# Score products of a retention kernel: one row tile per head, or four tiles of 64 by 64

## The reference, cut to what matters

```python
def _attn_ref(q, k, v):                       # B=2, H=8, S=768, D=64
    gamma = 1.0 - 2.0 ** (-5.0 - np.arange(H))
    for t in range(S):
        state = gamma * state + einsum('bhd,bhe->bhde', k[:, :, t], v[:, :, t])
        y[:, :, t] = scale * einsum('bhd,bhde->bhe', q[:, :, t], state)

def _moe_ref(x, U, V, w_ch1, w_ch2):          # x (2, 768, 512), rank 32
    u = x + ((x^T @ U @ V))^T                  # mixing over the tokens
    return u + relu(u @ w_ch1) @ w_ch2         # 512 -> 2048 -> 512

def _moe2_ref(x, w_in, w_spatial, b_spatial, w_out):
    h = relu(x @ w_in); u, v = halves of h
    v_n = v normalised over its 512 channels
    return (u * (w_spatial @ v_n + b_spatial)) @ w_out
```

## Time and profile before

| | us |
|---|---|
| median of three executions (464.69 to 465.3) | 465.14 |
| the profiled execution: its time | 464.75 |
| its span in the trace | 462.7 |
| PE busy | 456.1 (99%) |
| DVE busy | 351.2 (76%) |
| ACT busy | 253.6 (55%) |
| POOL busy | 48.4 (10%) |

### The profile page before, as it was taken

One profiled execution on the slowest core, in us unless ns is written; L12 is line 12 of the kernel. 1 busy time (PEld: TensorE's weight loads), 2 busy tenths in 40 slices (PEclk: granted clock), 3 DMA queues, 4 the chain that ended last, 5 costly groups with the idle time before them and its releaser, 6 DMA issues.

```text
span 462.7 us, 8760 instructions
## 1 busy us (share of the span) xinstructions
PE 456.1 (99%) x3176; PEld 407.9 (88%) x3176; DVE 351.2 (76%) x773; ACT 253.6 (55%) x592; POOL 48.4 (10%) x52
## 2 busy tenths in 40 slices
PE   8999999999999999999999999999999999999997
PEld 5788888999999999888888999988888789999997
DVE  4888879968889988864855976775722998895785
ACT  2676846456677555743474655643523675554352
POOL 2278960000000000000100000000100001000000
PEclk9999999999999999999999999999999999999999
DMA  8999601334342432211220333302105002032003
GB/s 310 408 316 349 243 1 47 136 138 137 136 141 87 145 118 93 93 37 55 92 91 3 102 135 120 101 1 92 47 0 204 1 0 93 0 124 104 1 1 136
DMA packets 20889, 51.36 MB, mean 111 GB/s; under 512 B 1520, under 2 KB 3952, under 8 KB 19568
## 3 DMA queue, kind: packets, MB, share of 16 engines
q1 hardware_dynamic: 20432, 50.29, 31.0%
q10 hardware_dynamic: 416, 0.53, 0.3%
HBM read 47.66 MB, written 3.15 MB: 110 GB/s over the span
## 4 chain that ended last, share of the span: by engine, by line
PE 88%; POOL 3%; DVE 3%; DMA 3%; ACT 1%; issue 1%; SPq 0%; DVEq 0%; POOLq 0%
PE bank L1632 10%; PE bank L1630 10%; PE bank L1633 9%; PE bank L1613 8%; PE bank L1611 8%; PE bank L1614 8%; PE bank L1737 3%; PE bank L1738 3%; PE bank L1735 3%; PE bank L1671 2%; PE bank L1672 2%; PE bank L1670 2%; PE bank L1753 2%; DMA tab<-decay 2%; PE bank L1518 1%; DMA att<-attn 1%
## 5 line engine op out<-in xcount | busy, mean ns | idle before, releaser
L1611 PE MATMUL bank<-bh,w1c 128*128 128x256 f32 x336 | 94.7, 282 | 0.1
L1614 PE MATMUL bank<-bh,w1c 128*128 128x256 f32 x336 | 94.7, 282 | 0.0
L1613 PE MATMUL bank<-bl,w1c 128*128 128x256 f32 x336 | 94.6, 282 | 0.0
L1632 PE MATMUL bank<-hl,w2h 128*128 128x512 f32 x192 | 75.9, 395 | 0.0
L1630 PE MATMUL bank<-hh,w2h 128*128 128x512 f32 x192 | 75.8, 395 | 0.0
L1633 PE MATMUL bank<-hh,w2l 128*128 128x512 f32 x192 | 74.7, 389 | 0.0
L1611 PEld LDWEIGHTS bank<-bh,w1c 128*128 128x128 f32 x336 | 63.5, 189 | 6.8 <-issue 0.4
L1102 DVE TENSOR_TENSOR c<-bank,p 128x256 f32<-128x256 f32 x72 | 30.5, 424 | 51.2 <-PE bank L1614 30.2
L1613 PEld LDWEIGHTS bank<-bl,w1c 128*128 128x128 f32 x336 | 63.4, 189 | 5.5
L1614 PEld LDWEIGHTS bank<-bh,w1c 128*128 128x128 f32 x336 | 63.4, 189 | 0.0
L683 ACT ACTIVATE p<-bank 128x256 f32<-128x256 f32 x72 | 27.6, 384 | 45.9 <-PE bank L1614 44.8
(11 more groups left out here) (180 smaller groups left out, 945.6 us busy)
## 6 DMA issues: line engine op xcount, KB each, us to landing
w1raw<-w SPq DMA_DIRECT2D x24, 512.0 KB, 5.1
w2raw<-w SPq DMA_DIRECT2D x24, 512.0 KB, 3.9
att<-attn SPq DMA_DIRECT2D x7, 1152.0 KB, 7.0
att<-attn SPq DMA_DIRECT2D x10, 384.0 KB, 5.2
out_T<-stage SPq DMA_DIRECT2D x7, 384.0 KB, 2.5
wsp_raw<-w_sp SPq DMA_DIRECT2D x1, 2304.0 KB, 8.2
winraw<-w_in SPq DMA_DIRECT2D x4, 512.0 KB, 5.0
tab<-decay SPq DMA_DIRECT2D x7, 258.0 KB, 4.2
```

What stands on the lines that cost most here:

```text
L1611: mm(o, w1c[k][:, 0, q, s], bh[:, q, c, :], start=(opens and c == 0), stop=False, skip_group_check=True)
L1613: mm(o, w1c[k][:, 0, q, s], bl[:, q, c, :], start=False, stop=False, skip_group_check=True)
L1614: m = mm(o, w1c[k][:, 1, q, s], bh[:, q, c, :], start=False, stop=(c == 1), skip_group_check=True)
L1632: mm(ch_ps[c][:, :], w2h[h][:, s], hl[k][:, h, :], start=False, stop=False, skip_group_check=True)
```

## The change

A score product of a head and a chunk, 128 keys by 128 queries with 64 head dimensions, is written as two products of 64 keys by 128 queries. Each takes 64 columns of the weights (keys) and writes 64 partitions of the head's bank. The two heads are the two row tiles as before, the two halves of the keys are now two column tiles, and the loop goes over heads inside and over halves outside. A group has 12 products of 64 x 64 tiles in the place of 6 of 64 x 128; the columns that stream through (128 queries) stay as many in each. Nothing else differs: what the banks hold, the waits, the one signal behind the last product, and the order of all other instructions are the same.

```diff
                 for c in range(G):
                     if i == 0 and g == 0 and c == 1:
                         pe.wait_ge(qk_group, 16)
-                    for a in range(2):
-                        r = slice(a * DH, (a + 1) * DH)
-                        t = slice((g * G + c) * P, (g * G + c + 1) * P)
-                        m = mm(sc_ps[a][:, c * P:(c + 1) * P], att[k][r, 1, t], att[k][r, 0, t],
-                               start=True, stop=True)
+                    t = (g * G + c) * P
+                    for j in range(2):
+                        w = slice(j * DH, (j + 1) * DH)
+                        for a in range(2):
+                            r = slice(a * DH, (a + 1) * DH)
+                            m = mm(sc_ps[a][w, c * P:(c + 1) * P], att[k][r, 1, t + j * DH:t + (j + 1) * DH],
+                                   att[k][r, 0, t:t + P], start=True, stop=True)
                 m.then_inc(sc_done, 1)
```

## The result

The changed kernel is measurably slower: 466.89 us in the median (14 executions) against 465.17 us for the kernel before (14 executions). The ratio is 1.0047, with a 95% interval of 1.0036 to 1.0058. One execution of the changed kernel, 499.24 us at a granted clock of 0.853, was in the slower state that single executions fall into and is left out of the ratio. The ratios of this document lie near those of the means (467.30 over 465.18 us here) and not of the medians, so single long executions weigh more in them. In a later comparison the same kernel had 466.70 us and a ratio of 1.0039 [1.0025, 1.0053]. The forecast was 465.3 us, no change that a measurement can tell. The time lies inside the forecast's range (464.5 to 467.2), but at the end that Rival 2 had opened, and the sign is the one that had 0.21.

A forecast was written before the change was run, and what follows sets the result against it. PE, busy 99% of the span, was taken as the bound. Items 3 and 4 at 0.10 us each, item 5 at 0 + g, sum to +0.19 us: 465.14 becomes 465.3 us, range 464.5 to 467.2.

The forecast's parts named there:

- Rival 2: Score groups: four tiles overlap but start slower, 0.040 us a record, slot 0.16 us; 2.1 us more, 467.2 us; chance 0.07.
- four tiles share the array: Score groups: four tiles run side by side, still 6 slots a group; 0.926 us in the place of 0.94.
- slot: Pitch at which a score group's sets of tiles follow each other: 0.112 us before, 0.117 us forecast, bounds 0.108 and 0.125.
- Rival 1: Score groups: the four tiles do not all overlap, 12 slots, 1.56 us a group; 472.8 us in all; chance 0.13.
- `kv`'s pace for a record: 0.029 us a record in the `kv` products, taken for the changed scores as nearest form; gives 0.117 us for four.
- the new form change: Transposes after each first score group now wait, as the tile form differs: load 0.07 us before scores' end, not 0.28; +0.18 us.
- g: Change in one score group's time against 0.94 us: forecast -0.014 us, bounds -0.06 and +0.03.
- g + 0.11: Items 3 and 4: delay of ACT's copy L641, and DVE and `down` with it; +0.10 us in each item.
- Rival 3: Score groups: a real gain, slots of 0.055 us, g of -0.34; -0.8 us, 464.3 us; chance 0.02.
- The second group goes straight into the path: g: Item 5: the second score group's change counts in full on the path that leaves for POOL; -0.014 us.
- Nothing behind 63 us changes: After the changed stage: that part is bound by its own products, so it adds nothing to the sum.
- the chain up to 19.54 us: Start of the kernel: the chain that ended last hangs on DMAs there (12.21 + 7.33 us).

The follow-up runs named there:

- firstg: Four tiles only in the first score groups of items 1 to 7, against the kernel before, 24 instructions more an item: 465.27 us, ratio 1.0003.
- second: Four tiles only in the second score groups of items 2 to 7, against the kernel before, 24 instructions more an item: 465.23 us, ratio 1.0000.
- after_relief: Changed kernel with only q loaded for items 5 and 6 and the second w2raw load issued behind the loop: 465.22 us, ratio 0.9999.
- before_light: Kernel before with only q loaded for item 6, which is computed with item 4's keys and values: 465.21 us, ratio 0.9998.

## Why the prediction was right or wrong

**Right: four tiles share the array.** Forecast 0.926 us for a group, measured 0.89. The slot stays at 0.11 us, since the streamed columns set it, and Rival 1 (1.56 us) is out. The rule on row groups that stood for Rival 1 (the Trainium skill, "TensorE: Matmul & The Clock Gate", Part 3) is contradicted by the four records in 0.34 us. The small miss: `kv`'s pace for a record, 0.029 us, was taken for starting four. They start at `outputs`' slot or close to it, which was the forecast's lower bound.

**Right in item 3, and right by luck in the sum: the new form change.** The load was to stand 0.07 us before the scores' end, and it stands at 0.08. By the group measured, g is -0.05, so g + 0.11 = 0.06 us for each of items 3 and 4. In the trace `down` stood 0.50 us late in item 3 (30.95 against 30.45 us), 0.06 more than the start's 0.44. In item 4 it stood 0.78 us late (38.21 against 37.43), 0.28 more. There the transposes waited for DVE's `u_add`, a wait that the forecast did not have:

```profile
36.01 0.59 PE L1535 MATMUL bank<-ident,xT 64*128 64x64 f32 x12 [0.16 <-DVE u L1044]
```

Item 5, forecast at 0, gave 0.22 us back, since PE had waited there before (its second scores are 0.55 us late). The two misses cancel, and 0.11 us are left for a forecast of 0.20 with the larger group. `firstg` shows the same form changes to cost too little to be measured.

**Right: no gain.** A group shorter by 0.05 us gave none that can be measured: `second` has 1.0000, `after_relief` 0.9999. Rival 3's short slots are not there.

**Wrong: item 5's term in the sum, "The second group goes straight into the path: g".** With g = -0.014 us it priced the group's 12 records more at the array's pace alone and had no term for bringing their instructions. In the profiled execution this group lasted 2.40 us in the place of 1.10, +1.30 us, with 1.15 us of it in one gap at a block's border, and all of it went through POOL to the end. In the medians the term that was missing measured 466.70 to 466.89 less 465.22 us (`after_relief`), some 1.5 to 1.7 us, eight times the forecast's whole sum. "Nothing behind 63 us changes" held: the products at 73.43 us are 1.85 us late, and the span is 1.8 us longer. Rival 2 named PE's instruction fetch in one sentence, gave its price to another mechanism (a slower start of each record, 467.2 us) and its chance as 0.07. Its time came out nearly right, but its mechanism was not there: groups without a gap last 0.89 us, where it needed 1.14. That the measured time lies inside the range is luck, since the upper end stood for this rival. The failure is one of reading. The view of DMA queues had the instruction queue, 26 packets for the whole program, which gives the size of a block, and the timeline had one group of 1.10 us among groups of 0.94. I took 0.94 as the price of all of them and never asked what the hole was.

**Wrong: the chain up to 19.54 us.** I read it as hanging on DMAs. DVE's step for `vst` (L1181) began at 18.74 us in the kernel before, ahead of that landing, and the start moved with PE's work in the changed kernel's profile. It cost the forecast nothing: the median of `item0`, with the change in item 0 alone, shows no loss.

**Right, as a test**: POOL's L530 was to start at about 45.6 us and a shift of the next stage's products by more than 0.5 us was to make the forecast wrong. They came at 47.28 us and with +1.85 us, and this pointed at item 5 at once.

**What stays open.** Lighter loads remove the gaps, and the gaps end 1.3 to 1.5 us after a packet lands. Why the packet before a gap starts as late as 5.8 us after PE has passed a border, and whether it waits behind data in the DMA engines or in memory, no run here separates. `after_relief` lightens three loads at once, so the share of each is not known, and only one of the three has its control in the kernel before (`before_light`). A gain of the other two by themselves is not excluded by a run; against it, the profile of `after_relief` has no shorter span than before (463.2 against 462.7 us), and its median is that of the kernel before.

## What to carry to other kernels

A change that makes more and smaller instructions of the same work has a price beside the engine's time: count the instructions of a stage and look when each packet of the instruction queue lands and whether PE still has more than some 1.5 us of work up to the block's border then. Here that failed where the DMA engines were 0.95 busy and a block lasted 6.6 us of work. Where a group of identical instructions lasts longer once than elsewhere, with nothing waited for, look for a block's border before taking the shorter one as its price. Tiling in both dimensions gave nothing here, where the tiles filled the array before. Where it must be, a stage in which the DMA engines have room is the place to try it; no run here did.

## What the runs showed of the hardware

- PE stops at borders 256 instructions apart when the next block comes late, for 0.6 to 1.8 us in seven profiled executions, and goes on 1.3 to 1.5 us after the packet landed. The profile has no releaser for it and says "issue".
- With lighter loads in the DMA queue the same block's packet started 1.5 us after the border before, in the place of 5.8 us, and no gap was left.
- A gap of 1.78 us (37.53 to 39.31 us) was followed by a granted clock of 0.50 at 41 to 43 us, and the span was 467.2 us, where the same kernel with a gap of 1.15 us had 464.5. One late block can so cost more than itself.
- Four 64 x 64 tiles run side by side at the slot of two 64 x 128 tiles, 0.11 us for 128 fp32 columns.
- Transposes of fp32: six of 128x128 take 0.88 us, twelve of 64x128 in two row tiles 0.54 us.
